# Linear attention under a two-layer expert network: the order of TensorE's attention tasks within a chunk

## The reference, cut to what matters

```python
# attention, for each step t
m_new = np.maximum(f_gate[:, :, t] + m, i_gate[:, :, t])
C = f_stab[:, :, None, None] * C + i_stab[:, :, None, None] * np.einsum('bhd,bhe->bhde', vt, kt)
n = f_stab[:, :, None] * n + i_stab[:, :, None] * kt
h_tilde = np.einsum('bhde,bhe->bhd', C, qt)
y[:, :, t] = o * h_tilde / np.maximum(np.abs(nq), 1.0)
# first network
h = x @ w_in
g = np.maximum(h, 0.0) + alpha * np.minimum(h, 0.0)
x = g @ w_out
# second network
h = np.maximum(np.maximum(x @ w1, x @ w2), x @ w3)
out = h @ w_out
```

## Time and profile before

| | us |
|---|---|
| median of three runs (785.97 to 787.31) | 786.6 |
| the profiled execution's own time | 786.5 |
| its span in the trace | 784.7 |
| TensorE busy | 736.7 (94%) |
| VectorE busy | 478.2 (61%) |
| ScalarE busy | 310.1 (40%) |
| GpSimd busy | 184.3 (23%) |

### The profile page before, as it was taken

The page is one execution under the profiler, slowest core; times in us unless marked ns, Lnnn a source line. Parts: engine busy times, 40 slices in busy tenths (PEclk is TensorE's granted clock), DMA queues, the critical chain, the costliest instruction groups (busy, mean ns, idle before and its releaser), DMA issues.

```text
span 784.7 us, 11547 instructions
## 1 busy us (share of the span) xinstructions
PE 736.7 (94%) x4410; PEld 653.6 (83%) x4410; DVE 478.2 (61%) x823; ACT 310.1 (40%) x648; POOL 184.3 (23%) x187
## 2 busy tenths in 40 slices
PE   2556999999999999999999999999999999999997
PEld 2545999999998888888888888888888888888886
DVE  6455888878978886888688754934242432434222
ACT  4453455456355444644554345421211212121211
POOL 4266533334525332434233200000000000000000
PEclk9866999999999999999999999999999999999999
DMA  6971232323123221331020054030110202000000
GB/s 195 284 215 53 75 99 78 101 71 114 61 78 107 77 96 43 110 102 65 34 63 0 1 176 130 1 112 2 36 40 0 74 1 74 0 34 1 34 0 34
DMA packets 40057, 56.37 MB, mean 72 GB/s; under 512 B 3457, under 2 KB 29058, under 8 KB 39618
## 3 DMA queue, kind: packets, MB, share of 16 engines
q1 hardware_dynamic: 39570, 54.57, 22.4%
q10 hardware_dynamic: 432, 1.06, 0.4%
HBM read 47.65 MB, written 7.96 MB: 71 GB/s over the span
## 4 chain that ended last, share of the span: by engine, by line
PE 83%; DVE 7%; POOL 3%; DMA 3%; SPq 2%; issue 1%; ACT 1%; ACTq 0%; DVEq 0%; POOLq 0%
PE bank L666 25%; PE bank L630 20%; PE bank L644 5%; PE bank L646 5%; PE bank L645 5%; PE bank L556 4%; PE bank L680 3%; PE bank L681 3%; PE bank L682 3%; PE bank L648 2%; PE bank L649 2%; PE bank L564 1%; PE bank L571 1%; POOL wproj L371 1%; DMA u_bcast<-u_scratch 1%
## 5 line engine op out<-in xcount | busy, mean ns | idle before, releaser
L630 PE MATMUL bank<-x_split,w_hi 128*128 128x512 f32 (+2 forms) x560 | 168.8, 369 | 2.2 <-ACT x_split L762 2.2
L630 PE MATMUL bank<-x_split,w_lo 128*128 128x512 f32 (+2 forms) x336 | 120.9, 362 | 0.0
L630 PEld LDWEIGHTS bank<-x_split,w_hi 128*128 128x128 f32 x560 | 103.6, 191 | 14.9 <-ACT x_split L762 2.6
L798 ACT ACTIVATE g_full<-bank 128x512 f32<-128x512 f32 (+2 forms) x112 | 59.7, 533 | 137.0 <-PE bank L630 136.1
L996 DVE SCALAR_TENSOR_TENSOR g_full<-g_full,beta,bank 128x512 f32<-128x512 f32 (+2 forms) x112 | 74.6, 666 | 34.6 <-ACT g_full L798 34.1
L644 PE MATMUL bank<-g_hi,wproj 128*128 128x512 f32 (+2 forms) x224 | 84.6, 378 | 5.2 <-DVE g_lo L977 5.2
L807 ACT ACTIVATE g_hi<-g_full 128x512 fp32r<-128x512 f32 (+2 forms) x112 | 63.2, 564 | 64.0 <-DVE g_full L996 63.9
L1017 DVE TENSOR_TENSOR best<-bank,first_of_max 128x512 f32<-128x512 f32 x36 | 24.9, 691 | 102.5 <-PE bank L666 76.1
L977 DVE TENSOR_TENSOR g_lo<-g_full,g_hi 128x512 fp32r<-128x512 f32 (+2 forms) x112 | 70.2, 627 | 18.9 <-ACT g_hi L807 18.1
L646 PE MATMUL bank<-g_hi,wproj 128*128 128x512 f32 (+2 forms) x224 | 81.0, 362 | 0.0
L645 PE MATMUL bank<-g_lo,wproj 128*128 128x512 f32 (+2 forms) x224 | 80.8, 361 | 0.0
(11 more groups left out here) (115 smaller groups left out, 1399.3 us busy)
## 6 DMA issues: line engine op xcount, KB each, us to landing
u_bcast<-u_scratch SPq DMA_DIRECT2D x24, 512.0 KB, 4.1
kv<-in_kv SPq DMA_DIRECT2D x24, 324.0 KB, 3.0
out<-final SPq DMA_DIRECT2D x6, 640.0 KB, 3.8
q_t<-in_q_t SPq DMA_DIRECT2D x24, 120.0 KB
k_t<-in_k_t SPq DMA_DIRECT2D x48, 60.0 KB
wproj_raw<-in_w_out SPq DMA_DIRECT2D x4, 640.0 KB, 9.9
o_gate<-in_o_gate SPq DMA_DIRECT2D x4, 640.0 KB, 4.9
w_raw<-in_w_max SPq DMA_DIRECT2D x2, 1152.0 KB, 6.3
```

The source lines that it names most:

```text
L630: ins = pe.matmul(ps[:, 0:cols], w[:, a, f], xs[:, x, 0:cols], start=(m == 0), stop=(m == 7))
L798: act.activation(gf[:, n % GF_SLOTS, 0:cols], hid[j % HID_BANKS][:, 0:cols], ACT.Relu, scale=-1.0).then_inc(neg_done, 1)
```

## The change

`chunk_groups` is rewritten. TensorE's tasks of a chunk stood at three places with network work between them: scores of ch, then carried part and state of ch, then values of ch. Now one group holds the values of ch and, right behind, the scores, the carried part and the state of ch+1. VectorE's part of a chunk is cut finer: taking prob's rest is a step of its own (`rest`), and the folding of carried part and state is another (`fold`), each in a later group than the matmuls that it reads. GpSimd's split of the rest moves with `rest`; its decaying of the state stays with `carry`, and so now comes ahead of that split. The gates of chunk ch+2 (ScalarE) come behind `pack` of ch+1; those of ch+1 had stood with the values and the finish of ch. In `first_plan` the two gates of chunk 3 are added, behind `prepare 3` and ahead of `turn 0` and `turn 1`. The ring keeps its three banks. No instruction is added or taken away, but for where the trace merges them.

```diff
--- before.py
+++ after.py
@@ -71,21 +71,23 @@
 
 def first_plan():
 
-    steps = [("prepare", 0), ("prepare", 1), ("gate", 0, 0), ("gate", 0, 1), ("scores", 0), ("carry", 0),
+    steps = [("prepare", 0), ("prepare", 1), ("gate", 0, 0), ("gate", 0, 1), ("scores", 0), ("carry", 0), ("fold", 0),
              ("gate", 1, 0), ("gate", 1, 1), ("values", 0), ("scores", 1), ("finish", 0, 0), ("finish", 0, 1),
-             ("prepare", 2), ("carry", 1), ("values", 1), ("gate", 2, 0), ("gate", 2, 1), ("pack", 2, 0),
-             ("finish", 1, 0), ("finish", 1, 1), ("pack", 2, 1), ("prepare", 3)]
+             ("prepare", 2), ("carry", 1), ("fold", 1), ("values", 1), ("gate", 2, 0), ("gate", 2, 1), ("pack", 2, 0),
+             ("finish", 1, 0), ("finish", 1, 1), ("pack", 2, 1), ("prepare", 3), ("gate", 3, 0),
+             ("gate", 3, 1)]
     return steps + [("turn", 0), ("turn", 1)]
 
 
 def chunk_groups(ch):
 
     more, later = ch + 1 < NCH, ch + 2 < NCH
-    return [[("scores", ch)], [("carry", ch)],
-            [("values", ch)] + more * [("gate", ch + 1, 0)],
-            more * [("gate", ch + 1, 1)] + [("finish", ch, 0)],
-            [("finish", ch, 1)] + more * [("pack", ch + 1, 0)] + later * [("prepare", ch + 2)],
-            more * [("pack", ch + 1, 1)]]
+    first = [[("scores", ch), ("carry", ch)], [("rest", ch)], [("fold", ch)]] if ch == PLAIN else []
+    return first + [[("values", ch)] + more * [("scores", ch + 1), ("carry", ch + 1)],
+                    more * [("rest", ch + 1)] + [("finish", ch, 0)],
+                    more * [("fold", ch + 1)] + [("finish", ch, 1)],
+                    more * [("pack", ch + 1, 0)] + later * [("prepare", ch + 2)],
+                    more * [("pack", ch + 1, 1)] + later * [("gate", ch + 2, 0)], later * [("gate", ch + 2, 1)]]
 
 
 def block_plan(b):
@@ -910,11 +912,13 @@
                         heads = slice(g * HG, (g + 1) * HG)
                         dve.tensor_tensor(prob[:, heads, :], ps[:, :].rearrange("p (k t) -> p k t", k=HG),
                                           ub[:, c, heads, :], ALU.mult).then_inc(prob_done, 1)
-                        if ch >= PLAIN:
-                            dve.wait_ge(prob_done, NG * ch + g + 1)
-                            dve.tensor_tensor(prob_r[:, heads, :], prob[:, heads, :], high(prob[:, heads, :]),
-                                              ALU.subtract).then_inc(prob_rest, 1)
-                if kind == "carry":
+                if kind == "rest":
+                    for g in range(NG):
+                        heads = slice(g * HG, (g + 1) * HG)
+                        dve.wait_ge(prob_done, NG * ch + g + 1)
+                        dve.tensor_tensor(prob_r[:, heads, :], prob[:, heads, :], high(prob[:, heads, :]),
+                                          ALU.subtract).then_inc(prob_rest, 1)
+                if kind == "fold":
                     ps = ring[TASKS.index(("carry", ch)) % RING_BANKS]
                     dve.wait_ge(carry_out, ch + 1)
                     wait(dve, inner_in, NG * ch)
@@ -1127,7 +1131,7 @@
                         pool.wait_ge(v_mid, n + 1)
                         pool.tensor_tensor(v_parts[:, :, 2, 0:D], v_r[:, :, :], v_parts[:, :, 1, 0:D], ALU.subtract
                                            ).then_inc(v_packed, 1)
-                if kind == "scores" and ch >= PLAIN:
+                if kind == "rest":
                     for g in range(NG):
                         pool.wait_ge(prob_rest, NG * (ch - PLAIN) + g + 1)
                         heads = slice(g * HG, (g + 1) * HG)
```

## The result

| | before | changed |
|---|---|---|
| median (lowest to highest), us | 786.3 (785.5 to 787.3) | 860.1 (859.4 to 862.0) |
| ratio, 95% interval | | 1.094 (1.092 to 1.097) |
| span of the profiled execution, us | 784.7 | 858.9 |

The account below looks back on a forecast made before the run. TensorE, busy for all 77 us of a 512-column block, was taken to set the time; 2.0 + 10.8 + 2.2 + 1.8 + 0.8 - 2.6 = 15.0 on top of 786.5 gave 801.5 us, range 790 to 815.

Parts of the forecast that it names:

- Cost A: In the joined group behind H0, the fourth task waits 0.4 us for VectorE's first reduction; five blocks, 2.0 us.
- Cost B: In the joined group behind H4, ScalarE's exponentials delay the first reduction; TensorE waits 2.7 us in blocks 2 to 5: 10.8.
- Cost C: In the joined group behind H11 (blocks 2 to 4, 0.6 us each) and block 1's H10 (0.4): together 2.2 us.
- the ring's waits: Six tasks on three banks: the group's fourth task waits until VectorE's first reduction has drained the first task's bank.
- The start: Block 0: H0 begins 4.9 us late, covered by TensorE's wait for GpSimd; decay ahead of the split adds 0.8 us.
- Gain: Chunks 2 to 23: 43 fewer returns from attention at 0.08 us, less the seams from values to scores: 2.6 us.
- cost B's clock: Times counted from the group's start in block 4, step by step per engine, ending in a 2.7 us wait behind H4.
- it just fits: P1 in block 4 needs VectorE's L977 of H1 at 11.8 us; that ends at 11.55, so no wait.
- D: P1 in the 384-column blocks 1 and 2 waits 0.9 us for L977, behind rests and finish: 1.8 us.
- rival of crowding: VectorE and GpSimd lengthen each other's instructions: 1.0 us more ahead of each of 13 groups, 814.5 us; chance 0.13.
- sign of being wrong: Wrong if the forecast reduction waits are missing, TensorE mostly waits for something else, or block 4 takes under 79 us.
- the granted clock at 1.00: Inside the blocks, TensorE's waits of up to a few us were taken not to lower its clock: nothing.

## Why the prediction was right and wrong

- **Cost A**, 0.4 us behind H0 in five blocks: 0.4 in blocks 3 to 5, as forecast, and 0.1 in blocks 1 and 2.
- **Cost B**, 2.7 behind H4 in four blocks, 10.8: 0.5, 2.7, 2.7 and 1.4 in blocks 2 to 5, 7.3 in all. Right to the tenth in two blocks; in block 4 the chain of ScalarE behind it was shown by taking the loads away. In block 2 a network step is shorter, and in block 5 TensorE itself came later, at a low clock.
- **Cost C**, 0.6 behind H11 of blocks 2 to 4 and 0.4 behind H10: 0.1, 1.4 and 1.4, and 0.1. Undersized in the 512-column blocks: in block 4 the finish beside GpSimd had held up L1000, and ScalarE's g_hi waited 5.8 us for it (until 423.53).
- **Behind P3 and P5** the prediction had nothing. P3 of block 1 has the same exponentials with their table load ahead of it, and waits 1.6.
- **All the ring's waits together**: 13.5 us, where A, B and C have 15.0. The mechanism is right. That the sum comes so near is in part luck: B was put too high, C and P3 too low.
- **The start**, 0.8 with the 4.9 covered: 1.2 (69.70 against 68.47), covered. Right.
- **Gain**, 2.6: nothing. The prediction took each of three returns for a cost of 0.08. Only the one behind values is one, and the seam from values to scores inside the group costs the same; so a chunk costs as much joined as apart (4.15 us).
- **The step that failed** is in cost B's clock: "the finish's first part 1.67", and with it "P1 needs that L977 at 11.8: it just fits". It took its 1.67 from a row in which GpSimd was idle, and placed it right behind the rests, whose release of GpSimd's splits is the change itself. It took 4.4 there, in block 4, and P1 waited 2.8 us for that L977. The prediction had stretched the rests (0.6 and 1.0), the instructions that had shown it, and not those that came beside GpSimd anew. This turned zeros into two waits for g_lo of 2.5 to 2.7 us by the list in each of blocks 3 and 4, and made D, 0.9 in blocks 1 and 2, 2.0 and 3.6 there. Its rival of crowding had the mechanism and a price of 1 us a group; the finish alone is 2.0 longer in the mean, up to 2.7. Its own sign of being wrong, that TensorE mostly waits for g_lo, is what came.
- **Second**: that waits "of up to a few us leave the granted clock at 1.00", taken as nothing. No row of before had shown it, and it does not hold here. From the clock column, (1 - clock) x length gives 3.4, 5.4, 1.8 and 1.8 us for blocks 1 to 4 and 1.6 for block 5, all zero before, and about 6 more in block 0 behind the values of chunk 2: at most some 20 of the 74 us, as a low clock during a wait costs nothing.
- **Third**: block 0. The sum had 0.8 for it and it grew by 17.7 besides the work that moved there, with three waits for g_lo of 3.5, 3.5 and 5.2. Of 256-column blocks the prediction said only that groups behind a P do not wait in the ring; it never laid VectorE's crowded queue against network steps half as long.

Added up from the trace: 35.6 us more of waits for g_lo, 13.5 in the ring, some 20 of clock and 1.2 at the start are 70 of the 74.2. The list counts each wait a little short (2.66 for 2.8 in block 4), which is some 2 more.

**What is left with both causes lessened.** In the variant with short split and early gates 24 us are left over the kernel before. Its granted clock in blocks 1 to 5 (columns: us, busy us and instructions of PE, PEld, DVE, ACT and POOL, then PEclk):

```profile
118.90:483.00 364.10, 351.66 (x2298) 312.04 (x2298) 257.46 (x500) 173.05 (x381) 93.50 (x121) 1.00 0.22 68
```

So it is not the clock there. Those blocks are 14 us longer, or 17 with the work that moved to block 0, and TensorE's list has 7.5 us for the last piece of v and 3.0 for g_lo; the short waits in the ring come to 4.8. Block 0 is 8.2 longer, 3.1 of it moved work. What stays open is how the 74 us divide between causes: the finish beside GpSimd, the gates' place and the clock that follows the waits overlap (7.6 us in common for the first two), and no run takes the low clock away and leaves the waits.

## What to carry to other kernels

When an edit moves instructions of two engines, list for each moved one what will run beside it on the other engine, and take its duration from a row with that neighbour, not from the row of before. If an engine is the one that is always busy, look for what it will wait for next before counting the wait that the edit adds: here the waits for g_lo, which the sum had at 1.8 us, grew by 35.6, while the ring's waits, on which most of its working went, came to 13.5 where it had 15.0. And give an off-path engine's work to idle time rather than to a later place: putting it off gained nothing, moving it into two idle stretches gained 0.8%.

## What the runs showed of the hardware

An instruction of VectorE on 8 elements a partition took 0.89 us instead of 0.17 when GpSimd's split was running, and an addition of 328 elements 1.34 instead of 0.50. Instructions with an operand in PSUM kept their length beside GpSimd: in the changed kernel, L1000 on 512 columns took 0.73 to 0.75 in all 64 rows, 12 of them wholly or partly beside GpSimd, and L927 0.53 to 0.55 in all 24, 9 of them so. The reciprocal (L960), with one input, took 0.20 also in the 11 rows beside GpSimd. That agrees with the Trainium skill (SBUF — State Buffer, Who interferes with whom): VectorE and GpSimd share a pair of ports, and of a GpSimd instruction and a VectorE instruction that has two SBUF inputs, or is in a mode with two ports, the one that comes second is blocked until the first is through. The finish was longer by 2.7 us for it in 11 of the 22 chunks and by 1.6 in nine.

The granted clock fell after a wait of 2.5 us at 387.8 to 390.3 but not after one of 2.7 at 379.2 to 381.9 in the same block; at the like place of block 5 (a wait of 2.7 that ends at 470.04) it was 0.79 over 466 to 474 us. A longer distance at a change of task is not always a cost. Read by single starts in the trace, the 16 passes of scores are 0.112 us apart, and so is the carried part's first from the last of them (c_pair_turns, 314.54 to 314.65): 1.79 in all. In the kernel before, the network's first matmul starts 0.03 behind the last pass, and its second 0.31 behind that, together what 0.11 and 0.23 would be. So coming back from scores costs nothing, and from the state neither (0.03 and 0.31 again). Behind values nothing is made up: 0.08 more show to the network's second matmul (0.31 for 0.23) and, in the joined group, to the second pass of scores (0.19 for 0.11; scores take 1.87 there). Putting the tasks next to one another saved nothing.
